# A wait for the last scattered rows on POOL, ahead of its end

## What is computed

```python
mask = q_assign[:, :, :, None] == k_assign[:, :, None, :]
scores = np.where(mask, scale * np.matmul(q, k.transpose(0, 1, 3, 2)), -1000000000.0)
attn = softmax(scores)
x = (attn @ v) as rows of 512
h = x @ w_in
x = (h * (1.0 / (1.0 + np.exp(-1.702 * h)))) @ w_out
noisy_logits = x @ w_gate + np.log1p(np.exp(x @ w_noise)) * noise
top2, top2_w = the two largest of each row, and their softmax
for e in range(E):
    for k in range(2):
        mask = top2[:, k] == e
        h = np.maximum(x[mask] @ w1[e], 0.0)
        out[mask] += top2_w[mask, k, None] * (h @ w2[e])
```

## Time and profile before

| | us |
|---|---|
| median of 3 runs | 917.96 |
| lowest, highest | 917.26, 921.13 |
| the profiled execution | 921.95 |
| its span, first to last instruction | 920.2 |
| PE busy | 897.9 (98%) |
| DVE, ACT, POOL busy | 528.1, 420.9, 143.6 |
| start of the last scatter on POOL | 912.99 |

### The profile page before, as it was taken

The page is one execution under the profiler, slowest core; times in us unless marked ns, Lnnn a source line. Parts: engine busy times, 40 slices in busy tenths (PEclk is TensorE's granted clock), DMA queues, the critical chain, the costliest instruction groups (busy, mean ns, idle before and its releaser), DMA issues.

```text
span 920.2 us, 12560 instructions
## 1 busy us (share of the span) xinstructions
PE 897.9 (98%) x4353; PEld 736.0 (80%) x4355; DVE 528.1 (57%) x959; ACT 420.9 (46%) x689; POOL 143.6 (16%) x147
## 2 busy tenths in 40 slices
PE   6999999999999999999999999999999999999995
PEld 4777777777776888888888888888888888888884
DVE  6688887887866444436443645644345343434383
ACT  4577767777668222344234323424434243433420
POOL 2021221221222000002300140500000000005073
PEclk8899999999999999999999999999999999999998
DMA  5123332331353323323532343625252544527464
GB/s 125 35 70 106 94 104 67 113 109 44 97 199 134 134 99 113 116 85 120 169 123 91 125 150 130 222 95 197 95 186 89 190 146 145 170 92 268 164 195 164
DMA packets 84302, 119.00 MB, mean 129 GB/s; under 512 B 19258, under 2 KB 47930, under 8 KB 84256
## 3 DMA queue, kind: packets, MB, share of 16 engines
q1 hardware_dynamic: 79328, 104.08, 35.1%
q0 software_dynamic: 4928, 14.35, 4.5%
HBM read 89.12 MB, written 29.39 MB: 129 GB/s over the span
## 4 chain that ended last, share of the span: by engine, by line
PE 78%; DVE 9%; issue 5%; POOL 4%; DMA 1%; ACT 1%; SPq 1%; POOLq 0%; DVEq 0%; ACTq 0%
PE psum L818 10%; PE psum L902 9%; PE psum L904 9%; PE psum L903 9%; PE psum L917 8%; PE psum L919 8%; PE psum L918 8%; PE psum L783 3%; PE psum L803 3%; PE psum L804 3%; DVE neg_max L1432 2%; POOL got L647 2%; POOL acc L647 1%; DVE recip L1456 1%; PE psum L915 1%
## 5 line engine op out<-in xcount | busy, mean ns | idle before, releaser
L818 PE MATMUL psum<-probs,vx 128*128 128x386 f32 x384 | 156.4, 489 | 0.4 <-ACT probs L1141 0.4
L917 PE MATMUL psum<-down_hi,hid_hi 128*128 128x512 f32 x384 | 151.1, 393 | 0.7 <-DVE hid_lo L1704 0.7
L919 PE MATMUL psum<-down_hi,hid_lo 128*128 128x512 f32 x384 | 149.9, 390 | 0.0
L918 PE MATMUL psum<-down_lo,hid_hi 128*128 128x512 f32 x384 | 149.9, 390 | 0.0
L1311 ACT ACTIVATE hid_hi<-psum 128x448 fp32r<-128x448 f32 x64 | 35.0, 546 | 180.4 <-PE psum L904 180.4
L1141 ACT ACTIVATE probs<-psum 128x384 f32<-128x384 f32 x192 | 90.5, 489 | 55.9 <-PE psum L804 53.3
L1432 DVE TENSOR_REDUCE neg_max<-psum 128x1 f32<-128x768 f32 x96 | 91.3, 955 | 25.8 <-PE psum L783 22.2
L1745 DVE SCALAR_TENSOR_TENSOR hid_lo<-psum,hid_hi 128x384 fp32r<-128x384 f32 x64 | 35.6, 556 | 117.4 <-ACT hid_hi L1311 117.4
L1284 ACT ACTIVATE gelu<-psum 128x512 f32<-128x512 f32 x48 | 28.7, 598 | 157.2 <-PE psum L904 157.2
L803 PE MATMUL psum<-qa,ka 102*128 102x384 f32 x192 | 93.9, 489 | 0.6 <-DVEq L1445 0.5
L903 PE MATMUL psum<-sx_lo,up_hi 128*128 128x448 f32 x256 | 93.5, 365 | 0.0
(11 more groups left out here) (208 smaller groups left out, 1548.1 us busy)
## 6 DMA issues: line engine op xcount, KB each, us to landing
raw<-in_moe_w SPq DMA_DIRECT2D x64, 512.0 KB, 4.2
raw<-in_moe_w_in SPq DMA_DIRECT2D x24, 512.0 KB, 3.5
raw<-in_moe_w_out SPq DMA_DIRECT2D x24, 512.0 KB, 5.1
slot_x<-zeros SPq DMA_DIRECT2D x7, 1024.0 KB, 5.6
slot_rows<-slot_x SPq DMA_DIRECT2D x8, 768.0 KB, 6.7
raw_q<-in_q SPq DMA_DIRECT2D x30, 192.0 KB, 3.3
raw_k<-in_k SPq DMA_DIRECT2D x30, 192.0 KB, 3.7
slot_y<-y_sb SPq DMA_DIRECT2D x7, 768.0 KB, 3.6
```

The lines of the kernel that those rows point to most:

```text
L818: mm(psum[:, 5 + half, 0:WIDE], vx[:, n % 2, c], probs[:, at % SLOTS], start=(c == 0), stop=(c == J - 1)).then_inc(unit_done, 1)
L917: mm(dst, hid_hi[:, held, cols], down_hi[:, slot, f % GP], start=(f == 0), stop=False)
L918: mm(dst, hid_hi[:, held, cols], down_lo[:, slot, f % GP], start=False, stop=False)
L919: return mm(dst, hid_lo[:, held, cols], down_hi[:, slot, f % GP], start=False, stop=(f == pieces - 1))
```

## The change

```diff
@@ -704,6 +704,7 @@
                     out=out, out_offset=bass.IndirectOffsetOnAxis(ap=end_row[0:rows_of(j), j:j + 1], axis=0),
                     in_=y_sb[0:rows_of(j), j], in_offset=None, bounds_check=N - 1, oob_is_err=False)\
                     .then_inc(finished, DMA)
+            pool.wait_ge(finished, DMA * YT)
             pool.wait_ge(rounds_ready, 1)
             more = pool.value_load(more_rounds[0:1, 0:1], min_val=0, max_val=ROUNDS - 1)
             with pool.If(more > 0):
```

## The result

The changed kernel takes 923.49 us (median of 20 runs, 920.30 to 924.66), the kernel before in the runs beside it 918.75 us (median of 20, 917.26 to 922.06). The ratio is 1.0039 with a 95% interval of 1.0029 to 1.0049: **slower by 3.6 us, 2.7 to 4.5**. The two medians lie further apart, 4.7 us, because the 20 times of the kernel before fall into two groups (11 from 917.3 to 918.8, 9 from 919.6 to 922.1) and the median stands at the edge of the lower one; the means, 919.4 and 923.1, are 3.7 us apart. The prediction was +3.0 us. Its absolute figures (921.0, range 914.8 to 923.0) were set against a median of 917.96 from three runs; with the 20 of before the median is 0.8 us higher, and the changed kernel's median is 4.7 us above that one, so 923.49 itself lies 0.5 us above the range. The difference added to the old median, 917.96 + 3.6 = 921.6, lies inside it.

The account below looks back on a forecast made before the run. It took matmuls to fill nearly the whole span and POOL's closing DRAIN to set its end. A DRAIN of 5.96 us less 2.95 gave +3.0 us on 917.96, so 921.0 us, range 914.8 to 923.0.

Parts of the forecast that it names:

- What sets the end: End of the block (L121): POOL's DRAIN of 7703 ns sets the end, and the last 3.9 us after SP has finished.
- (a): At the new wait: POOL stands until `finished` is full, seen within hundredths of SP's 916.0 us.
- (b): Behind the wait: register load, short instructions and branch, 0.98 us, lose their cover, so the DRAIN is issued at 916.98.
- (c): Other engines: they meet POOL only at the closing barrier; SP's waits, matmuls and transfers keep their times.
- (d): End of the span: the new end differs from the old by D - 2.95 us; D was taken as 5.96 us, chance 0.42.
- D: POOL's last DRAIN: the time it takes when everything has landed already; taken as 5.96 us, break-even 2.95 us.
- The reading of the ordinary waits: Earlier waits on POOL (such as L669): POOL goes on within 0.6 us, leaving no room for 3.93 us of clearing up.
- The sum: Whole kernel: 5.96 - 2.95 = +3.0 us, giving 921.0 us, 0.33% slower.
- The whole 7.70 again: Rival on POOL's last DRAIN: it costs its whole length again, +4.75 us, 922.7 us; chance 0.15.
- The 3.93: Rival on POOL's last DRAIN: its work begins only after the last landing, +1.0 us, 918.9 us; chance 0.15.
- The short DRAIN: Rival on POOL's last DRAIN: about 0.05 us once all has landed, -2.9 us, 915.1 us; chance 0.20.

Follow-up runs that it names:

- e5: The changed kernel with the wait for `finished` put behind the read of `more_rounds` instead of ahead of it; one run, 925.15 us.
- e6: The changed kernel with 24 more small plain transfers (16 rows of 16 bytes) on POOL at about 601 us and a wait for their landing; one run, 930.29 us.
- e7: The changed kernel with 24 more large transfers (128 rows of 2 KB) on POOL at about 601 us and a wait for their landing; one run, 928.63 us.
- e1: The kernel before with one more DRAIN on POOL at about 601 us, behind the loads of end_meta; one run, 918.01 us.
- e2: The changed kernel with two more DRAINs on POOL, at 601 us and behind the gathers to `acc` (about 851 us); 918.94 us, ratio 0.9991 to before.
- e8_after: The changed kernel measured again, without further edits; median 923.37 us, ratio 1.0040 to the kernel before.
- e3: The kernel before, without the new wait, with one more DRAIN on POOL behind the gathers to `slot_rows` (about 901 us); ratio 0.9971 to before.

## Why the prediction was right

- **What sets the end.** Right: POOL's DRAIN. Taking it away from the end brings 2.7 us of run time (3.8 us by the profile).
- **(a) The wait ends with SP's.** Right: SP's branch and POOL's load both stand at 915.3.
- **(b) 0.98 us laid bare.** Right: the DRAIN starts at 916.3, 1.0 us after the landing. e5 takes 0.8 of it back by putting the load under the scatters again.
- **(c) Nobody else waits for it.** Right: the scatters keep their 5.3 us, and SP's DRAIN stands 0.2 us behind its branch as before.
- **(d) D = 5.96 us.** Measured 5.953. It was the choice between 3.93, 5.96 and 7.70, and its reason held too: 72 transfers at 83 ns (82 measured), worked off after POOL's last preparation and beside the last landing. e6 and e7 showed that it is the count, e1 and e2 that it can be worked off earlier. A part of the agreement is luck: the 5.96 us behind the preparation equal D only because in the kernel before the first half (2.95 us) outlasted the landing (2.0 us). In e1 the same reading would have given 3.1 us for a DRAIN of 32 transfers, for which the line above has 2.7. The reading of the ordinary waits, that POOL goes on at once and does no clearing up there, held in e6 and e7: POOL waited for the 24 transfers, and paid for them at the end all the same.
- **The sum.** +3.0 us, and from SP's branch to the end the profiles show 4.2 and 7.2. The intervals of the measured +3.6 and +3.7 take it in. The 0.6 us above it have no cause shown. One part can move: the wait costs what lies between preparation and landing plus the 0.98, and that first part was 2.0 us in the profile of before, 1.8 in the changed kernel's and 2.6 in e8_after's, which puts the price at 3.0, 2.8 and 3.6 us. The prediction took the 2.0 us of one execution for all.
- **The rivals.** The whole 7.70 again: no, 1.74 us of it were waiting for POOL's own scatters, and there the row speaks against what the Trainium skill (Perfetto Trace Analysis, "Sequencer-only Instruction (DRAIN, etc)") says, that such an instruction's time in the profile holds no waiting; the 21.4 us of e3's late DRAIN do so more plainly. The 3.93: no. The short DRAIN: no for 72 transfers. The 12 ns that the Trainium skill (VectorE: DVE Perf Modes, "The DRAIN you can't avoid") gives are for the DRAINs that the runtime puts ahead of a kernel and behind it; this one is the kernel's own, at the end of its block, and took 5.95 us on POOL, so the prediction leant on a figure for another DRAIN. But the rival has its place, which the prediction didn't see: with 4 transfers left it is 0.39 us, and a wait ahead of it costs little more than the 0.98 us of the load.

## What to carry to other kernels

An engine that issues transfers by its own program may have to account for each of them at the end of its block, as POOL does here, and a wait for their landing doesn't do that work: it only sets it back behind the landing. Before adding a wait ahead of an instruction, ask what that instruction does in the shadow of what is waited for; here 3.0 us lay there. Put such an account where the engine idles (here ahead of the last four transfers), and move reads that depend on nothing, such as the load of a loop count, to the near side of the wait.

## What the runs showed of the hardware that I had not expected

- POOL's DRAIN takes 50 ns + 82 ns for each transfer that POOL issued since its last DRAIN: 0.389 us for 4, 1.686 for 20, 5.953 for 72, 7.985 for 96, the same for transfers of 0.2 KB and 256 KB, and long after they landed.
- With transfers in flight, about 41 ns for each transfer since the last DRAIN came after the last landing (n = 4, 16, 32, 40, 68), and the profile counts the waiting into the DRAIN's time (21.4 us at most).
- A DRAIN on POOL in an idle stretch clears the account and puts off nothing: 2.7 us less for one line in each of two comparisons (0.9971), which makes this version faster than both kernels.
- The first of the last four scatters isn't alike in all versions: with the late DRAIN it starts 0.37 us later behind DVE's first result and takes 1.08 us instead of 1.45, and both end at the same time. It is not the late DRAIN alone: in e2, which has DRAINs only at 601 and 851 us, it takes 1.12 us.
